# Attention units of 128 queries with 64-key windows in place of tiles of 64 queries with 96 keys, inside a fused attention and mixture-of-experts kernel

## The chip, the cores and the metric

The kernel runs on one core of one Trainium2 chip. The metric is device time in microseconds (us) of one launch. PE is TensorE (matmuls), DVE is VectorE, ACT is ScalarE, POOL is GpSimd, SP is the engine that issues all DMAs here.

## The reference

Chunked attention, then a gated MLP, then a soft mixture of experts, all in float32:

```
q, k, v: (4, 8, 768, 64); mem_k, mem_v: (4, 8, 8, 64)
for each chunk c of 32 queries:
    keys = 8 memory keys + keys from 16 before the chunk to 8 behind it, cut at the ends of the sequence
    scores = (q_c @ keys.T) / 8; a = softmax(scores, max subtracted, sum + 1e-9)
    out[c] = a @ values
x = out as (3072, 512)
h = x @ w_in (512 x 2048); g = h * sigmoid(h); x = g @ w_out
logits = x @ phi (32 slots); dispatch = softmax over all 3072 tokens; slot_input = dispatch.T @ x
slot_out = relu(slot_input @ w1[e]) @ w2[e] for 8 experts of 4 slots
result = softmax(logits over the slots) @ slot_out
```

## The kernel before

The 3072 tokens are worked on in seven blocks of 256, 512 x 5 and 256 tokens (TILES counts them in tiles of 64). In block b PE runs 16 chunks k of the MLP (pe_mlp, 12 matmuls of 128x128 weights by 512 tokens, or 256 in the two short blocks, into one of two h_ps buffers), and between the chunks it does the attention of the tokens of block b+1 and the mixture's sums of block b-1. So the attention of block 1 runs within block 0, and that of block 0 ahead of everything (the start). PE's order is written out by hand in pe_block; act_block and dve_block have the same steps for ACT and DVE, and each engine works its own list strictly in order, with semaphores between them.

A tile of attention is 64 queries of 8 heads. S_STEP gives the chunks behind which its steps start; T_LAG and V_LAG say how many chunks later the next steps come:

- S, pe_scores: 8 matmuls of 64 queries by the tile's 96 keys (88 around the two query chunks and 8 memory keys). dve_scores scales them, adds a mask of -3e38 for keys that a query may not see (masks, from PSUM to sc in SBUF), and takes the maximum. act_exp does 4 exponentials of 96 keys with the maximum as bias and the sum in the accumulator. dve_rinv takes the reciprocals, and POOL multiplies sc by them.
- T, pe_probs_T: 4 transposes to pt_ps; act_pt copies them to pt.
- V, pe_values: 8 matmuls of the values by pt into o_ps. dve_x splits the result into a high part (fp32r) and a low part, which are the MLP's input x.

The names of the other steps on PE: L is pe_logits (once per four chunks of the MLP), then pe_fold and D, pe_dispatch (64 matmuls of 32x32 weights, once per block, behind chunk 4, or 5 in the last block); pe_w2 and pe_w2_T run once in block 0. keep_busy matmuls fill waits of PE at the start and the end.

Behind a chunk, ACT does the tanh of the gate (act_tanh) and DVE multiplies (dve_g) and transposes (dve_gb). Chunk k waits for dve_g of chunk k-2. The weights w_in are split too: ACT makes the high half wh (act_wh), POOL (the first two DVE) the low half wl (low_part); eight pieces in all, and in block 0 the chunks 4, 8 and 12 wait for two more pieces each (wl_done). After the last block come the slots' MLP over 32 units of expert weights that SP streams in, and the output.

In the matmul groups of the trace a float32 matmul leaves two records, an fp32r one and a transpose one record. SP loads a tile's q and k (320 KB) and v (192 KB) into a ring of four.

Of the kernel before, what the change touches and what calls it, by code (L numbers as in the profile page):

```python
# [7 lines left out]
QT = 64  # L8
# [9 lines left out]
PAIRS = H // 2  # L18
QKW = PAIRS * QT + PAIRS * KEYS
LOADW = QKW + H * D  # L20
RING = 4
SB = 3
# [4 lines left out]
TILES = (4, 8, 8, 8, 8, 8, 4)  # L27
NB = len(TILES)
LAST = NB - 1
FIRST = [sum(TILES[:b]) for b in range(NB + 1)]  # L30
NT = FIRST[-1]
TOKS = [QT * t for t in TILES]
TMAX = max(TOKS)
BATCH_TILES = S // QT

S_STEP = (0, 1, 6, 7, 8, 9, 10, 11)
T_LAG, V_LAG = 2, 3
# [4 lines left out]
W_FIRST = (1, 2)  # L42
W_NEXT = (0, 1, 3, 4, 6, 7)
W_LOW_BEFORE = {4: (2, 3), 6: (4, 5), 7: (6,), 8: (7,)}


def tile_at(b, k, lag):

    if b == LAST or k - lag not in S_STEP[:TILES[b + 1]]:
        return None  # L50
    return FIRST[b + 1] + S_STEP.index(k - lag)


def moe_program(nc, qk, v, w_in, w_outT, w_out, phi, w1, w2, out):
# [5 lines left out]
    with ExitStack() as ctx:  # L60
# [30 lines left out]
        masks = at("masks", R, [128, 3, KEYS])  # L91
        sc = at("sc", R + 288, [128, SB, PAIRS, KEYS])
        pt = at("pt", R + 288 + 1152, [KEYS, PAIRS, 2 * QT])
        row_stats = at("row_stats", R + 1952, [128, 4, SB, PAIRS])
        ring = at("ring", R + 2000, [128, RING, LOADW])
        assert 2000 + RING * LOADW <= 4 * HALF_W
        nmax, rsum, rinv = (row_stats[:, i, :, :] for i in range(3))
# [18 lines left out]
        def x_of(b):  # L116
            return x_short if TILES[b] == 4 else (x_even, x_odd)[b % 2]

        def gt_of(b, k):
            if b == 0:  # L120
                return gT_short[:, k, :] if k < 2 * GT_RING else acc_short[:, k - 2 * GT_RING, :]
            return gT[:, (NCH * (b - 1) + k) % GT_RING, 0:TOKS[b]]

        def gb_of(b, k):
            if TILES[b] == 4:
                return gB_short[:, k, :]
            return gB[:, k + 16 if b % 2 and k < 8 else k, :]

        def gb_groups(b, i, j):

            rows, cols = slice(32 * i, 32 * i + 32), slice(32 * j, 32 * j + 32)
            if TILES[b] == 4:
                return gB_short[rows, :, cols]
# [13 lines left out]

        qk_in = [sem(f"qk_in{t}") for t in range(RING)]
        v_in = [sem(f"v_in{t}") for t in range(RING)]
# [23 lines left out]
        def q_of(n, p, h2):  # L173
            return ring[64 * h2:64 * h2 + 64, n % RING, p * QT:(p + 1) * QT]

        def k_of(n, p, h2):
            o = PAIRS * QT + p * KEYS
            return ring[64 * h2:64 * h2 + 64, n % RING, o:o + KEYS]

        def half_of(p, h2):  # L180

            return h2 ^ (p % 2)

        def v_of(n, h):
            return ring[0:KEYS, n % RING, QKW + h * D:QKW + (h + 1) * D]

        def s_of(n):
            return sx_ps if n >= TILES[0] or n % 2 == 0 else lpu_ps
# [6 lines left out]
        def pe_scores(pe, n, dispatched=0):  # L195
            pe.wait_ge(qk_in[n % RING], 16 * (n // RING + 1))
            if n >= TILES[0]:
                pe.wait_ge(sc_done, n)
            elif n >= 2:
                pe.wait_ge(sc_done, n - 1)  # L200
            if dispatched:
                pe.wait_ge(acc_done, 4 * dispatched - 1)
            for p in range(PAIRS):
                for h2 in range(2):
                    r, cols = 64 * half_of(p, h2), slice(p // 2 * KEYS, (p // 2 + 1) * KEYS)
                    last = nc.tensor.matmul(s_of(n)[r:r + 64, p % 2, cols], q_of(n, p, h2), k_of(n, p, h2),  # L206
                                            start=True, stop=True)
# [716 lines left out]
```

## Time and profile before

| | us |
|---|---|
| median of 3 runs | 522.82 (521.74 to 528.11) |
| profiled execution | 526.73 |
| its span, first to last instruction | 524.9 |
| PE busy | 492.9 (94%) |
| DVE busy | 306.2 (58%) |
| ACT busy | 181.2 (35%) |
| POOL busy | 55.8 (11%) |

Busy time says how long an engine had an instruction under way. For PE it is modelled, and a PE that is always busy can still spend its time in short gaps between unlike matmuls. A stage's length is read from the starts of its instructions. The execution and its span differ by 1.8 us; the profiled execution was 3.9 us longer than the median of the runs.

### The profile page before, as it was taken

What the parts mean: (1) busy time and instruction counts of PE and PEld (TensorE: products, weight loads), DVE (VectorE), ACT (ScalarE), POOL (GpSimd) and SP (SyncE); (2) the same over time, 40 slices, a digit from 0 to 9 for tenths busy, and PEclk for the clock granted to TensorE, in tenths of its full rate; (3) what the DMA queues carried; (4) which work ended last, traced back from release to release, by engine and by line L of the source; (5) the groups of instructions that cost most, each with busy time, mean ns of one, the idle gap of its engine ahead of it and who ended that gap; (6) DMA issues with size and microseconds to landing.
All of it is one profiled execution on the core that took longest, in us unless ns stands there. A gap on an engine that the chain in (4) does not pass through costs nothing.

```text
span 524.9 us, 11609 instructions
## 1 busy us (share of the span) xinstructions
PE 492.9 (94%) x4794; PEld 350.0 (67%) x4794; DVE 306.2 (58%) x733; ACT 181.2 (35%) x591; POOL 55.8 (11%) x65
## 2 busy tenths in 40 slices
PE   5779899999999999999999999999999989999972
PEld 4668677777776777776777767776677769643541
DVE  3546745756576676475665767656765466561222
ACT  3555623345333254341642505524132112110112
POOL 2154400011100011010110101101010000000000
PEclk9799999999999999999999999999999999999978
DMA  8587621202312013111132010341005659989997
GB/s 270 179 278 242 199 84 40 83 1 81 121 41 81 2 66 123 57 44 39 42 121 81 23 59 23 101 131 70 2 1 198 259 197 420 426 345 423 425 345 253
DMA packets 25125, 78.42 MB, mean 149 GB/s; under 512 B 2416, under 2 KB 8688, under 8 KB 19440
## 3 DMA queue, kind: packets, MB, share of 16 engines
q1 hardware_dynamic: 25072, 77.67, 41.1%
q8 instruction: 38, 0.62, 0.5%
q14 instruction: 15, 0.12, 0.1%
HBM read 71.37 MB, written 6.29 MB: 148 GB/s over the span
## 4 chain that ended last, share of the span: by engine, by line
PE 85%; DMA 8%; DVE 2%; ACT 2%; issue 1%; POOL 1%; SPq 1%; DVEq 0%; ACTq 0%
PE h_ps L243 52%; PE o_ps L225 6%; DMA unit<-w 5%; PE pt_ps L215 5%; PE lpu_ps L257 5%; PE sx_ps L206 4%; PE lpu_ps L277 3%; PE sx_ps L277 2%; DMA w_stage<-w_in 2%; PE h_ps L857 1%; PE h_ps L794 1%; DMA ring<-qk 1%; PE pt_ps L794 1%; ACT sc L352 1%; PE lpu_ps L265 1%
## 5 line engine op out<-in xcount | busy, mean ns | idle before, releaser
L243 PE MATMUL h_ps<-x_odd,wh 128*128 128x512 f32 x384 | 130.7, 402 | 0.0
L340 ACT ACTIVATE gT<-h_ps 128x512 f32<-128x512 f32 (+1 forms) x108 | 57.7, 534 | 154.9 <-PE h_ps L243 145.1
L352 ACT ACTIVATE sc<-sc,row_stats 128x96 f32<-128x96 f32 x192 | 69.7, 364 | 79.1 <-DVE row_stats L395 79.1
L422 DVE SCALAR_TENSOR_TENSOR gT<-gT,h_ps 128x512 f32<-128x512 f32 (+1 forms) x108 | 65.9, 610 | 53.1 <-ACT gT L340 51.4
L243 PE MATMUL h_ps<-x_even,wh 128*128 128x512 f32 x256 | 87.6, 403 | 0.0
L243 PEld LDWEIGHTS h_ps<-x_odd,wh 128*128 128x128 f32 x384 | 72.1, 188 | 23.1 <-issue 5.4
L243 PE MATMUL h_ps<-x_odd,wl 128*128 128x512 f32 x192 | 75.1, 391 | 0.0
L669 POOL TENSOR_TENSOR sc<-sc,row_stats 128x384 f32<-128x384 f32 x48 | 39.7, 827 | 324.8 <-DVE row_stats L402 324.8
L243 PEld LDWEIGHTS h_ps<-x_even,wh 128*128 128x128 f32 x256 | 48.0, 188 | 14.9 <-issue 3.4
L432 DVE STREAM_TRANSPOSE gB<-gT 128x512 f32<-128x512 f32 x80 | 56.6, 708 | 1.3
L243 PE MATMUL h_ps<-x_short,wh 128*128 128x256 f32 x256 | 54.3, 299 | 1.5 <-DVE gT L422 1.5
L243 PE MATMUL h_ps<-x_even,wl 128*128 128x512 f32 x128 | 50.1, 391 | 0.0
L243 PEld LDWEIGHTS h_ps<-x_short,wh 128*128 128x128 f32 x256 | 42.9, 197 | 7.6 <-issue 3.8
L243 PEld LDWEIGHTS h_ps<-x_odd,wl 128*128 128x128 f32 x192 | 36.1, 188 | 6.2
L225 PEld LDWEIGHTS o_ps<-pt,ring 96*64 96x64 f32 x768 | 27.2, 141 | 16.7 <-issue 16.3
L346 ACT COPY pt<-pt_ps 96x512 f32<-96x512 f32 x48 | 27.8, 579 | 29.0 <-PE pt_ps L215 24.2
L215 PE MATMUL pt_ps<-ident,sc 128*96 128x128 f32 x192 | 31.1, 286 | 6.2 <-POOL sc L669 4.2
L243 PE MATMUL h_ps<-x_short,wl 128*128 128x256 f32 x128 | 37.0, 289 | 0.0
L352 ACT ACTIVATION_READ_ACCUMULATOR sc<-sc,row_stats 128x1 f32 x192 | 35.9, 187 | 0.0
L225 PE MATMUL o_ps<-pt,ring 96*64 96x64 f32 x768 | 33.8, 232 | 1.9 <-DVE x_short L411 1.1
L215 PEld LDWEIGHTS pt_ps<-ident,sc 128*96 128x96 f32 x192 | 20.2, 129 | 19.1 <-issue 12.0
L389 DVE SCALAR_TENSOR_TENSOR sc<-sx_ps,masks 128x192 f32<-128x192 f32 x92 | 28.4, 350 | 5.9 <-PE sx_ps L206 5.9
(143 smaller groups left out, 567.8 us busy)
## 6 DMA issues: line engine op xcount, KB each, us to landing
unit<-w SPq DMA_DIRECT2D x32, 1024.0 KB, 11.4
ring<-qk SPq DMA_DIRECT2D x48, 320.0 KB, 3.1
ring<-v SPq DMA_DIRECT2D x48, 192.0 KB, 3.2
w_stage<-w_in SPq DMA_DIRECT2D x4, 1024.0 KB, 10.0
wot<-w_outT SPq DMA_DIRECT2D x4, 1024.0 KB, 8.1
unit<-w_out SPq DMA_DIRECT2D x4, 1024.0 KB, 5.7
out<-unit SPq DMA_DIRECT2D x4, 1024.0 KB, 7.4
out<-unit SPq DMA_DIRECT2D x2, 512.0 KB, 5.5
```

What stands on the lines that cost most here:

```text
L215: last = nc.tensor.transpose(pt_ps[0:KEYS, p * 128:(p + 1) * 128], sc[:, n % SB, p, :], ident[:])
L225: last = nc.tensor.matmul(o_ps[64 * h2:64 * h2 + 64, p * QT:(p + 1) * QT], v_of(n, 2 * p + h2), pt[:, p, QT * half_of(p, h2):QT * half_of( ...
L243: last = nc.tensor.matmul(h_ps[k % 2][:, 0:TOKS[b]], w[:, n, kc, q * 128:(q + 1) * 128], x[:, lo, kc, 0:TOKS[b]], start=(kc == 0 and w is ...
L257: last = nc.tensor.matmul(lp_ps[32 * q:32 * q + 32, 0:TOKS[b]], w2c[:, q, 32 * n:32 * n + 32], gt_of(b, 4 * n + q), start=(n == 0), stop=( ...
L277: last = nc.tensor.matmul(u_ps[i][32 * c:32 * c + 32, :], eB[32 * i:32 * i + 32, 32 * j:32 * j + 32], gb_groups(b, i, j), start=(r == 0), ...
L340: nc.scalar.activation(gt_of(b, k), h_ps[k % 2][:, 0:TOKS[b]], ACT.Tanh, scale=0.5).then_inc(tanh_done, 1)
L346: nc.scalar.copy(pt[:], heads(pt_ps[0:KEYS, :])).then_inc(pt_done, 1)
L352: last = nc.scalar.activation(sc[:, i, p, :], sc[:, i, p, :], ACT.Exp, bias=nmax[:, i, p:p + 1], accum_out=rsum[:, i, p:p + 1])
L389: last = nc.vector.scalar_tensor_tensor(out=sc[:, i, c::2, :], in0=s_of(n)[:, c, 0:2 * KEYS].rearrange("p (a k) -> p a k", a=2), scalar=D ...
L422: nc.vector.scalar_tensor_tensor(out=gt_of(b, k), in0=gt_of(b, k), scalar=1.0, in1=h_ps[k % 2][:, 0:TOKS[b]], op0=ALU.add, op1=ALU.mult).t ...
L432: nc.vector.transpose(gb_of(b, k), gt_of(b, k)).then_inc(gb_done, 1)
L669: nc.gpsimd.tensor_tensor(p, p, rinv[:, n % SB, :].unsqueeze(2).to_broadcast([128, PAIRS, KEYS]), ALU.mult).then_inc(p_done, 1)
```

## The change

- The work comes in units of 128 queries (24 of them; UNITS is 2, 4 x 5, 2). A query chunk of 32 gets its own window of 64 keys, WIN = 16 + 32 + 8 + 8, which it sees in full. The memory keys are placed within the 96 keys (key_order) so that both windows of a tile are contiguous. The masks are gone; at the two ends of a sequence dve_scores writes -3e38 over the columns outside it in PSUM.
- S is 32 matmuls of 32 queries by 64 keys, 8 of them at different places of the array in a row. DVE takes the maximum straight from PSUM and scales it; ACT takes 8 exponentials of 64 keys from PSUM with scale, bias and accumulator, 4 behind one chunk's tanh and 4 behind the next. The POOL multiply is over 512 columns instead of 384, and there is one per unit.
- T is 4 transposes of 128x128; ACT copies in two halves into pt, whose other places stay zero. V is 16 matmuls with 128 rows of weights, since v is loaded once per window (twice the overlap).
- ACT makes the high part of x (act_x), DVE the low part.
- There is one pause per four chunks: T behind chunk 0, 4, 8, 12 (1, 5, 9, 13 in block 0), then V, L and S behind the next one (V and S in block 0).
- q and k are loaded per unit (two in flight, freed by S), v per unit (three in flight). In the last block the gate's buffers are halved and doubled in number, D is behind chunk 6 and the logits behind 9, 10 and 13.
- In block 0 the pieces of wh are at chunks 2, 3, 6, 7, 10, 11 (W_NEXT), two per pause, and POOL's wl goes ahead of the multiply of the same unit (W_LOW_BEFORE). The start has longer keep_busy runs and includes the exponentials of unit 2.

```diff
+WIN = LEFT + CHUNK + RIGHT + NMEM
-TILES = (4, 8, 8, 8, 8, 8, 4)
-S_STEP = (0, 1, 6, 7, 8, 9, 10, 11)
-T_LAG, V_LAG = 2, 3
-W_NEXT = (0, 1, 3, 4, 6, 7)
-W_LOW_BEFORE = {4: (2, 3), 6: (4, 5), 7: (6,), 8: (7,)}
+UNITS = (2, 4, 4, 4, 4, 4, 2)
+W_NEXT = {2: 2, 3: 3, 6: 4, 7: 5, 10: 6, 11: 7}
+W_LOW_BEFORE = {3: (2, 3), 4: (4, 5), 5: (6, 7)}
+def values_at(b, n):
+    if b >= LAST or UNITS[b + 1] == 2 and n % 2 == 0:
         return None
+    return FIRST[b + 1] + (n if UNITS[b + 1] == 4 else n // 2)
+def scores_at(b, n):
+    return values_at(b, n + 1) if n < 3 else values_at(b + 1, 0)
+def pause(b):
+    return 2 if b == 0 else 1
...
+            for t in range(2):
+                for c in range(2):
+                    for p in range(PAIRS):
+                        for h2 in range(2):
+                            a, r = place_of(p, h2)
+                            at = (2 * t + c) * WIN
+                            last = nc.tensor.matmul(s_of(u)[32 * r:32 * r + 32, a, at:at + WIN], q_of(u, t, c, p, h2),
+                                                    k_of(u, t, c, p, h2), start=True, stop=True)
...
         def pe_block(pe, b):
             for k in range(NCH):
                 pe_mlp(pe, b, k)
+                n, at_pause = k // 4, k % 4 == pause(b)
+                if k % 4 == pause(b) - 1 and values_at(b, n) is not None:
+                    pe_probs_T(pe, values_at(b, n))
...
+                if at_pause and values_at(b, n) is not None:
+                    pe_values(pe, values_at(b, n))
...
+        def act_exp(act, u, a):
+            if a == 0:
+                act.wait_ge(nmax_done, u + 1)
+            for g in range(4 * a, 4 * a + 4):
+                last = nc.scalar.activation(sc[:, u % SB, g, :], by_window(u)[:, a, g - 4 * a, :], ACT.Exp, scale=D ** -0.5,
+                                            bias=rmax[:, u % SB, g:g + 1], accum_out=rsum[:, u % SB, g:g + 1])
...
+        def act_x(act, u):
+            hi, lo = unit_x(u)
+            act.wait_ge(o_mm, u + 1)
+            nc.scalar.copy(hi, heads(o_ps)).then_inc(xh_done, 1)
...
         def act_block(act, b):
             for k in range(NCH):
                 if b == 0 and k in W_NEXT:
-                    act_wh(act, 2 + W_NEXT.index(k))
+                    act_wh(act, W_NEXT[k])
                 act_tanh(act, b, k)
+                if k % 4 == pause(b) + 1 and scores_at(b, n) is not None:
+                    act_exp(act, scores_at(b, n), 1)
+                if k % 4 == pause(b) - 1 and values_at(b, n) is not None:
+                    act_pt(act, values_at(b, n))
+                if at_pause and values_at(b, n) is not None:
+                    act_x(act, values_at(b, n))
...
+                if at_pause and scores_at(b, n) is not None:
+                    act_exp(act, scores_at(b, n), 0)
```

PE in block 1, behind chunk 9, before: V (o_ps), L (w2c), T (pt_ps) and S (sx_ps) of three different tiles, between two chunks of the MLP (h_ps).

```order
L243 MATMUL h_ps<-x_odd,wh 128x512
L225 MATMUL o_ps<-pt,ring 64x64 x8
L257 MATMUL lpu_ps<-gT,w2c 32x512 x4
L215 MATMUL pt_ps<-ident,sc 96x128 x4
L206 MATMUL sx_ps<-ring 64x96 x8
L243 MATMUL h_ps<-x_odd,wh 128x512
```

The same place after the change.

```order
L261 MATMUL h_ps<-x_odd,wh 128x512
L242 MATMUL o_ps<-pt,v_sb 64x64 x16
L275 MATMUL lpu_ps<-gT,w2c 32x512 x4
L219 MATMUL sx_ps<-qk_sb 32x64 x32
L261 MATMUL h_ps<-x_odd,wh 128x512
```

The transposes have moved to a break of their own one chunk earlier; behind chunks 10 and 11, where before V, T and S of the next tiles follow each time, nothing stands any more.

ACT in block 0, chunks 4 to 7 before: wh is a piece of the weights, gT the tanh, sc the exponentials.

```order
L340 ACTIVATE gT<-h_ps 128x256 x2
L368 CAST wh<-w_stage 128x1024
L340 ACTIVATE gT<-h_ps 128x256
L352 ACTIVATE sc,row_stats<-sc,row_stats 128x96 x4
L368 CAST wh<-w_stage 128x1024
L340 ACTIVATE gT<-h_ps 128x256
L352 ACTIVATE sc,row_stats<-sc,row_stats 128x96 x4
```

ACT at chunks 5 to 7 after the change (x_odd is the high part of x, written by act_x).

```order
L375 COPY pt<-pt_ps 64x16x32 x2
L408 CAST wh<-w_stage 128x1024
L365 ACTIVATE gT<-h_ps 128x256
L394 CAST x_odd<-o_ps 128x4x128
L382 ACTIVATE sc,row_stats<-sx_ps,row_stats 128x64 x4
L408 CAST wh<-w_stage 128x1024
L365 ACTIVATE gT<-h_ps 128x256
L382 ACTIVATE sc,row_stats<-sx_ps,row_stats 128x64 x4
```

The second wh piece of a pause stands behind x and the first four exponentials of the unit scored in that pause; before, the pieces 2 and 3 stood at chunks 0 and 1, well ahead of chunk 4.

## Rows read from the trace of the kernel before

**Rows 1.** The page, part 1: PE's busy time.

```profile
PE 492.9 (94%) x4794; PEld 350.0 (67%) x4794; DVE 306.2 (58%) x733; ACT 181.2 (35%) x591; POOL 55.8 (11%) x65
```

**Rows 2.** Stretches: block 0; block 2; block 6; expert weights. Clock, DMA share last.

```profile
28.40:81.40 53.00, 45.94 (x528) 37.25 (x517) 30.40 (x89) 26.40 (x93) 18.33 (x13) 0.94 0.60 198
...
150.00:218.60 68.60, 68.60 (x646) 48.57 (x650) 45.25 (x105) 26.70 (x92) 6.62 (x8) 1.00 0.19 63
...
414.00:448.00 34.00, 32.45 (x355) 26.50 (x354) 20.73 (x49) 7.20 (x19) 0.00 (x0) 1.00 0.78 313
...
466.00:506.00 40.00, 36.10 (x450) 17.12 (x450) 12.30 (x33) 4.42 (x8) 0.00 (x0) 0.99 0.98 392
```

**Rows 3.** The chain that ended last, in order of time: start, us, what.

```profile
479.25 26.78 DMA unit<-w
```

**Rows 4.** Waits of PE in block 0: us in total, times, longest.

```profile
PE pt_ps L215 <- POOL sc L669: 4.2, 2, 3.5
```

**Rows 5.** Timeline of PE around S of one tile: start, us, what.

```profile
218.17 0.39 PE L243 MATMUL h_ps<-x_odd,wh 128*128 128x512 f32 x1
218.49 0.56 PE L206 MATMUL sx_ps<-ring 64*64 64x96 f32 x16
218.98 0.50 PE L243 MATMUL h_ps<-x_odd,wh 128*128 128x512 f32 x1
```

**Rows 6.** Timeline of PE behind chunk 10 of block 2: V, T, S, next chunk.

```profile
194.07 0.69 PE L225 MATMUL o_ps<-pt,ring 96*64 96x64 f32 x16
194.69 0.64 PE L215 MATMUL pt_ps<-ident,sc 128*96 128x128 f32 x4
195.26 0.56 PE L206 MATMUL sx_ps<-ring 64*64 64x96 f32 x16
195.75 0.50 PE L243 MATMUL h_ps<-x_even,wh 128*128 128x512 f32 x1
```

**Rows 7.** Timeline of PE in D of block 2, and the chunk behind it.

```profile
166.40 0.62 PE L277 MATMUL sx_ps<-gB,eB 32*32 32x512 f32 x2
166.41 0.62 PE L277 MATMUL lpu_ps<-gB,eB 32*32 32x512 f32 x2
...
167.50 0.63 PE L277 MATMUL lpu_ps<-gB,eB 32*32 32x512 f32 x2
167.53 0.62 PE L277 MATMUL sx_ps<-gB,eB 32*32 32x512 f32 x2
...
170.78 0.50 PE L243 MATMUL h_ps<-x_even,wh 128*128 128x512 f32 x1
```

**Rows 8.** Groups of instructions on ACT, POOL, DVE: busy, mean ns, idle before.

```profile
L352 ACT ACTIVATE sc<-sc,row_stats 128x96 f32<-128x96 f32 x192 | 69.7, 364 | 79.1 <-DVE row_stats L395 79.1
L346 ACT COPY pt<-pt_ps 96x512 f32<-96x512 f32 x48 | 27.8, 579 | 29.0 <-PE pt_ps L215 24.2 <-PE o_ps L225 4.8
L368 ACT CAST wh<-w_stage 128x1024 fp32r<-128x1024 f32 x8 | 8.3, 1039 | 1.9 <-DMA w_stage<-w_in 1.9
...
L669 POOL TENSOR_TENSOR sc<-sc,row_stats 128x384 f32<-128x384 f32 x48 | 39.7, 827 | 324.8 <-DVE row_stats L402 324.8
L416 POOL TENSOR_TENSOR wl<-w_stage,wh 128x1024 fp32r<-128x1024 f32 x6 | 14.2, 2369 | 11.0 <-ACT wh L368 11.0
...
L395 DVE TENSOR_REDUCE row_stats<-sc 128x4 f32<-128x384 f32 x48 | 26.6, 553 | 1.6
```

**Rows 9.** Timeline of PE: keep_busy at the start, and pe_w2 in block 0.

```profile
7.61 1.16 PE L794 MATMUL h_ps<-ident,fold 128*128 128x128 f32 x8
...
69.26 3.64 PE L287 MATMUL lpu_ps<-wot,part 128*32 128x512 f32 x32
```

**Rows 10.** Timeline of PE behind its longest wait.

```profile
38.43 1.12 PE L225 MATMUL o_ps<-pt,ring 96*64 96x64 f32 x16
39.49 1.09 PE L215 MATMUL pt_ps<-ident,sc 128*96 128x128 f32 x4
```

**Rows 11.** One stretch of block 0 behind that wait; granted clock third from the end.

```profile
38.40:40.60 2.20, 2.20 (x23) 2.02 (x23) 0.96 (x3) 0.38 (x1) 2.19 (x1) 0.50 0.12 33
```

More of the change, by code:

```diff
@@ L88, in moe_program @@
         cmax, csum, crinv = (csoft[:, i, :] for i in range(3))
[L91 to L97, printed above, removed]
+        sc = at("sc", R, [128, SB, 2 * PAIRS, WIN])
+        pt = at("pt", R + 1024, [128, 4 * PAIRS, QT])
+        row_stats = at("row_stats", R + 2048, [128, 3, SB, 2 * PAIRS])
+        qk_sb = at("qk_sb", R + 2112, [128, QK_RING, 2, QKW])
+        v_sb = at("v_sb", R + 2112 + QK_RING * 2 * QKW, [128, V_RING, 2, H * D])
+        assert 2112 + QK_RING * 2 * QKW + V_RING * 2 * H * D <= 4 * HALF_W
+        rmax, rsum, rinv = (row_stats[:, i, :, :] for i in range(3))
         x_odd = at("x_odd", R + 4 * HALF_W, [128, 2, KC, TMAX], fp32r)
@@ L201, in pe_scores @@
             if dispatched:
                 pe.wait_ge(acc_done, 4 * dispatched - 1)
[L203 to L207, printed above, removed]
-            last.then_inc(s_mm, 1)
-        def pe_probs_T(pe, n):
-            pe.wait_ge(p_done, n + 1)
-            if n:
-                pe.wait_ge(pt_done, n)
-            for p in range(PAIRS):
-                last = nc.tensor.transpose(pt_ps[0:KEYS, p * 128:(p + 1) * 128], sc[:, n % SB, p, :], ident[:])
-            last.then_inc(p_tr, 1)
@@ L342, in act_pt @@
-        def act_pt(act, n):
-            act.wait_ge(p_tr, n + 1)
-            if n:
-                act.wait_ge(o_mm, n)
-            nc.scalar.copy(pt[:], heads(pt_ps[0:KEYS, :])).then_inc(pt_done, 1)
-        def act_exp(act, n):
-            act.wait_ge(nmax_done, n + 1)
-            i = n % SB
-            for p in range(PAIRS):
-                last = nc.scalar.activation(sc[:, i, p, :], sc[:, i, p, :], ACT.Exp, bias=nmax[:, i, p:p + 1],
-                                            accum_out=rsum[:, i, p:p + 1])
-            last.then_inc(exp_done, 1)
+            r = NCH * (b - 1) + k
@@ new lines, in act_tanh, with act_pt @@
+            nc.scalar.activation(gt_of(b, k), h_ps[k % 2][:, 0:TOKS[b]], ACT.Tanh, scale=0.5).then_inc(tanh_done, 1)
+        def act_pt(act, u):
+            act.wait_ge(p_tr, u + 1)
+            if u:
+                act.wait_ge(o_mm, u)
+            else:
+                act.wait_ge(pt_zero, 1)
+            for c in range(2):
+                half = slice(64 * c, 64 * c + 64)
+                last = nc.scalar.copy(pt[half, :, c * CHUNK:(c + 1) * CHUNK], pt_ps[half, :].rearrange("p (j q) -> p j q", q=CHUNK))
+            last.then_inc(pt_done, 1)
@@ L506, in dve_block @@
                     dve_acc(dve, b - 1)
-        places = [(7, h_mm, NCH * LAST - NCH)] + [(i, o_mm, NT) for i in range(4)]
+        places = [(7, h_mm, NCH * LAST - NCH)] + [(i, o_mm, NUN) for i in range(4)]
         places += [(4, h_mm, NCH * LAST), (5, h_mm, NCH * LAST)]
@@ L662, in _ @@
                 pool.wait_ge(const_set, j + 2)
-            for n in range(NT):
+            for n in range(NUN):
                 for m in W_LOW_BEFORE.get(n, ()):
```

378 lines of the change are left out of this document (192 added, 186 removed).

## The prediction

> **What bounds the kernel now.** Three views, in this order. The page's first part has PE busy for 492.9 of 524.9 us [rows 1], so PE's own list sets the time, but an average does not say where. The stretches do: block 2 lasts 68.6 us with PE busy throughout at the full clock, DVE at 45.25 and ACT at 26.70 us [rows 2]. There what counts is PE's work and the gaps between unlike matmuls; a faster DVE is worth nothing. Block 0 is different: 53.0 us with 45.94 busy and a mean clock of 0.94. Its longest wait of PE is 3.5 us, for POOL's multiply of probabilities, which stood behind a piece of wl [rows 4]. Behind it the granted clock is 0.50, the level of 1.2 GHz [rows 11]. In block 6 PE is idle for 1.55 of 34.0 us. At the end the chain runs over DMA for 26.78 us [rows 3], the DMA engines being 98% busy from 466 to 506 us; those loads start when PE has finished earlier steps, so time won on PE ahead of block 6 moves them too and counts in full.
>
> **PE in a full block, step by step.** I call a pause's steps T, V, S, L and D as the code does.
>
> Breaks. With S alone, the last matmul of a chunk starts at 218.17, S at 218.49, the next chunk at 218.98 [rows 5]. The last matmul streams for 0.23 us (2.72 us per uninterrupted chunk by 12), so 0.09 is lost ahead of S; the first matmul behind a break takes 0.1 us longer than its neighbours. A break costs 0.2 us beside its content. Before, 15 of 16 chunks of a full block are followed by one; afterwards 9 (chunks 0, 1, 2, 4, 5, 8, 9, 12, 13). 6 x 0.2 = 1.2 us less.
>
> T. 194.69 to 195.26 is 0.57 us ahead of S [rows 6], 0.36 to 0.40 ahead of a chunk; the mean of 8 is 0.48, or 3.8 us per block. Afterwards four sets of four, with 128 columns for 96; nearest is a set of 128x128 transposes elsewhere in this trace at 0.46 us, so 1.8 us. 2.0 us less.
>
> V. 194.07 to 194.69 is 0.62 us for 8 matmuls, 16 records [rows 6]. Within it pairs start every 0.058 us, with 0.1 at the start and 0.15 at the end. A unit has 32 records: 0.1 + 15 x 0.058 + 0.15 = 1.13 us, in place of 1.24. 0.4 us less.
>
> S. This is the unknown price. Before, 0.49 us for 16 records of 96 keys, four at a time at the four places of 64x64. Afterwards 64 records of 64 keys, eight at a time. Low end: if only streaming counts, eight rounds of 0.058 and the ends, 0.65 us per unit. High end: D has 128 records of 32x32 places from 166.39 to 170.78 [rows 7], 0.034 us each, so 64 x 0.034 = 2.2 us. D also shows how it gets there: its first records start 0.007 us apart (two per row, rows 0.013 apart), later ones 0.017 apart (167.50 to 167.53 for two), with a gap of 0.19 us each 32 records. I take what D does as long as its queue is full, and the slower rate behind it: 32 records in four rounds, 0.11 + 3 x 0.058, then 32 x 0.017 = 0.54, and 0.26 for gap and ends, 1.1 us, against 2 x 0.49 before. 0.5 us more per block.
>
> Sum of a full block: -1.2 - 2.0 - 0.4 + 0.5 = -3.1, rounded with the restarts to -3.2 us. For blocks 1 to 4 that is -12.8, and -1.1 more since block 4 has three S instead of four. Block 5, with half the attention: 12 breaks become 7 (-1.0), T -1.0, V -0.2, S +0.3: -1.9.
>
> A rule speaks against this step. The Trainium skill (TensorEngine Tiling (Array Packing), Instruction Overhead) gives each small matmul some 60 cycles on trn2, and advises against tiling out of a dimension that is small already. At 2.4 GHz that is an estimate of 25 ns per record, 1.6 us for S. The trace has 7 and 17 ns between records of different places, so it does not agree for short runs. By the Trainium skill's figure the total would be near no change, since 21 units x 0.5 us take the whole gain.
>
> **Do the other engines keep up in a full block?** Take PE's S as ending at 0. DVE's maximum over 512 columns scales from 0.553 at 384 [rows 8] to 0.7, with the scaling 0.9 and the handover 0.2: 1.1. Four exponentials, 0.364 each [rows 8], 1.4: 2.5. The next chunk ends at 2.9 (with its fold 3.8), its tanh takes 0.6, the other four exponentials end at 5.0, the two DVE steps at 5.4, POOL's multiply (0.827 scaled by 512/384, 1.1) at 6.5. T is wanted behind the third chunk, at 8.3 or later. Its slack of 1.8 us is cover for all of ACT's added work, and x on ACT has the whole of the next chunk. Dropping the masks (0.35 us twice per tile) shortens DVE's list, which waits anyway: nothing. The larger v loads are hidden, with DMA at 0.19 in block 2 [rows 2]. No new wait, no gain.
>
> **Block 0.** Here the order of ACT makes a wait that was not there. From the start of T: T 0.46, chunk 1.5, V 1.1, S 1.1 end at 4.2. Maximum and scaling end at 5.4, exponentials (four) start at 5.6 and end at 7.0. Only then comes the second wh piece, 1.04 us [rows 8], to 8.0, since ACT works in order, and then POOL's wl, 2.37 [rows 8], to 10.4. The next chunk (4, 8 or 12) waits for that wl; its predecessor ended at 5.8. PE is idle for 4.6 us, with nothing beside it. Behind the ACT instruction stand also the tanh and the other exponentials; POOL's multiply is behind wl, but ends at 11.5, and T is wanted only at 13.5, behind two chunks of 1.5. So three periods of 13.5, 40.5 us.
>
> The first T of these: ACT bounds the start. First exponentials at 6.8 (as before; the q and k load is twice as large), 16 of them to 12.4. T waits for 20 keep_busy matmuls, 40 records at 0.145 [rows 9] = 5.8 us, to 15.3; the pt copies, 2 x 0.58 [rows 8] overlapping, 16.5; keep_busy and V 18.7; x, wh, pt 21.6; V of unit 1 22.8; x 24.7; maximum 25.6; eight exponentials 28.4; sums and multiply 29.9. Then 30 + 40.5 + 11.6 (T 0.5, w2 3.6 [rows 9], two chunks 3, V 1.1, S 1.1, transposes and logits 2.0, breaks 0.3) = 82.1, against 81.4 now [rows 2]. The low clock comes on top: after the 3.5 us wait of before, V took 1.06 instead of 0.62 and T 0.74 instead of 0.40 [rows 10], in all some 1.6 us. Three longer waits at 1.3 each, since part of the low stretch can fall into the wait: +4.0. Block 0 ends at 86.1: +4.7. Bounds: 0, if the wait is covered by less work ahead of wh than I count, and +9.
>
> **The last block and the tail.** D one chunk later, the ring of 12 buffers and the logits elsewhere: the transposes of dve_et still stand in front of a gate multiply, so the wait of 1.5 us stays; DVE's four sums now delay the gate behind D by some 0.6. +0.5. SP's queue for expert weights starts its long run at D, 1.4 us later; the DMA has about 2 us of air at 462 to 466, so it hides.
>
> **Sum.** -12.8 - 1.1 - 1.9 + 4.7 + 0.5 = -10.6 us. From the profiled execution, 526.73, that is 516.1; its runs' median is 3.9 us lower, 522.8, and I predict against that: 512.
>
> The Trainium skill (ScalarE: Activation LUTs, What ACT_TABLE_LOAD costs) gives 280 ns and 0.833 per element for an activation with a pointer as bias: 360 for 96 keys, and the row has 364, so it agrees. For 64 keys it is an estimate of 333, and block 0 and the start would be about 1 us shorter by it.
>
> **Rivals.**
> 1. Forecast: 512, between 509 and 516. Chance 0.42.
> 2. Block 0 costs nothing, or S runs near its low end. Without the +4.7: 507; with S at 0.65 as well, 21 units x 0.45 = 9.5 less, 498, but both together are unlikely. For it: four S records start within 0.02 us today. Against: the fixed order of ACT. About 507, chance 0.25.
> 3. A wait shows up in full blocks, or the low clock holds longer in block 0. If T waits 0.5 us per unit in 16 units, 8 us are gone: 520. Against it stands the slack of 1.8. Chance 0.19.
> 4. The other side: S is bound by its number of records all the way, as D is on average, at 2.2 us per unit. 21 units x 1.1 = 23 us more: 535. The gain is gone from 1.6 us per unit on, and it is 2% slower from 2.1. For it: twice as many records as before, and three quarters of D's run are at the slower rates. Against: V, S before and D's first 32 are far quicker. Chance 0.10, most of it below 2.1. The Trainium skill's estimate above (TensorEngine Tiling (Array Packing), Instruction Overhead) would put S at the first of these two points.
> 5. The change doesn't do what it says, the pauses being kept but lengthened by ring loads of q and k that come too late (two in flight, 640 KB each): about 522 to 535. Chance 0.04.
>
> **How the numbers follow.** A measurement of this kernel tells about 2%, 10.5 us, from no change: the line is at 512.4. Case 1 straddles it, slightly more below (0.23); with case 2 that is 0.48 for faster. Slower: 0.04 of case 4, 0.02 of case 5 and 0.02 of case 3: 0.08. Within 2%: 0.44. The range takes all of case 1, most of 2 and 3 and the lower part of 4: 503 to 521.
>
> **What would show it.** A full block of about 65.4 us instead of 68.6 with PE never idle; S of some 1.1 us between its start and the next chunk; T at 0.46, four per block. In block 0, three waits of PE of 4 to 5 us at chunks 4, 8 and 12, named after POOL's wl, with the clock at 0.50 behind each. The forecast is wrong if S takes 1.6 us or more, if T waits for POOL in full blocks, or if those three waits are absent or twice as long.

## The result, and the profile after

The changed kernel takes 504.39 us (median of four runs, 503.69 to 505.04) beside 524.17 for the kernel before on the same chip: a ratio of 0.962, interval 0.955 to 0.968. The forecast was 512, with 503 to 521 as its range. The sign is right, the time lies near the low end of the range, and the gain is nearly twice the one forecast. The profiled execution took 504.32 us (526.73 before, 2.6 above its median; so the profiles are 22.4 us apart and the medians 19.8). The page's first part, and then stretches of the changed kernel: block 0, block 2, block 6, and what follows the last block's matmuls.

```profile
PE 466.5 (93%) x5502; PEld 346.3 (69%) x5502; DVE 251.9 (50%) x508; ACT 182.6 (36%) x615; POOL 41.3 (8%) x41
```

```profile
22.70:83.90 61.20, 45.32 (x652) 39.60 (x652) 24.48 (x57) 29.73 (x111) 18.37 (x10) 0.86 0.49 178
144.50:207.90 63.40, 63.40 (x755) 47.27 (x754) 36.30 (x72) 26.84 (x95) 4.14 (x5) 1.00 0.22 76
...
392.60:427.00 34.40, 32.56 (x355) 26.43 (x354) 20.30 (x49) 7.20 (x19) 0.00 (x0) 1.00 0.89 361
427.00:502.50 75.50, 61.67 (x705) 33.05 (x703) 27.23 (x62) 10.68 (x21) 0.00 (x0) 0.96 0.96 380
```

PE is 26.4 us less busy than in [rows 1], with 708 more matmul records. A full block is still PE without a gap, now 63.4 us for 68.6 in [rows 2]. Block 0 went the other way: 61.2 us with 15.9 of them idle and a mean clock of 0.86.

Cut at the first MLP matmul of each block, the trace gives where the 22.4 us of span went:

```
                   before   after    change   forecast
start               26.49   22.72     -3.8  } together
block 0             54.82   61.21     +6.4  } +4.7
block 1             65.78   60.57     -5.2     -3.2
block 2             68.58   63.43     -5.15    -3.2
block 3             68.58   63.43     -5.15    -3.2
block 4             68.58   62.62     -6.0     -4.3
block 5             61.17   58.60     -2.6     -1.9
block 6             33.9    34.4      +0.5     +0.5
behind the matmuls  77.0    75.5      -1.4      0
sum                                  -22.4    -10.6
```

The waits of PE in block 0, as in [rows 4], are those forecast:

```profile
PE h_ps L261 <- POOL wl L458: 13.9, 3, 4.7
PE pt_ps L228 <- POOL sc L721: 1.8, 1, 1.8
```

The first of the three, in order of time; "<-" in brackets names what ended the idle time:

```profile
34.23 1.05 ACT L408 CAST wh<-w_stage 128x1024 fp32r<-128x1024 f32 x1
...
35.36 2.34 POOL L458 TENSOR_TENSOR wl<-w_stage,wh 128x1024 fp32r<-128x1024 f32 x1 [2.36 <-ACT wh L408]
...
37.76 0.58 PE L261 MATMUL h_ps<-x_short,wh 128*128 128x256 f32 x1 [4.60 <-POOL wl L458]
...
42.59 0.60 PE L228 MATMUL pt_ps<-ident,sc 128*128 128x128 f32 x4
```

ACT converts its second piece of wh behind the four exponentials, POOL's piece of wl follows, and chunk 4 starts with its end. The granted clock in the three stretches around these waits, third number from the end, is 0.50, the level of 1.2 GHz:

```profile
35.20:42.00 6.80, 4.25 (x20) 4.25 (x21) 2.71 (x6) 1.93 (x11) 3.38 (x2) 0.50 0.92 367
52.20:55.60 3.40, 2.90 (x13) 2.91 (x14) 0.98 (x3) 0.00 (x0) 1.48 (x2) 0.50 0.97 380
65.90:72.70 6.80, 5.51 (x26) 5.51 (x27) 2.33 (x5) 0.67 (x3) 2.28 (x2) 0.50 0.00 1
```

In a full block, the break behind chunk 1 of block 2, timeline of PE (compare [rows 6]):

```profile
150.52 1.15 PE L242 MATMUL o_ps<-pt,v_sb 128*64 128x64 f32 x32
151.60 1.06 PE L275 MATMUL lpu_ps<-gT,w2c 128*32 128x512 f32 x8
152.60 0.86 PE L219 MATMUL sx_ps<-qk_sb 64*32 64x64 f32 x64
153.38 0.50 PE L261 MATMUL h_ps<-x_even,wh 128*128 128x512 f32 x1
```

V takes 1.08 us (151.60 less 150.52). S, whose price was the large unknown, takes 0.78 for its 64 records, less than two of the old S. The last chain over the DMA engines has nearly the length that it had in [rows 3]; it starts 21 us earlier:

```profile
458.32 26.43 DMA unit<-w
```

### The profile page after: what moved, and what is told of

Same layout as the page of the kernel before. It is cut to its first block, busy times and chain, and to the rows that moved or that the text cites. A ratio compares the mean times of both kernels' runs of the same rounds, so it can differ in the third digit from the quotient of the medians.

```text
span 502.5 us, 12654 instructions
## 1 busy us (share of the span) xinstructions
PE 466.5 (93%) x5502; PEld 346.3 (69%) x5502; DVE 251.9 (50%) x508; ACT 182.6 (36%) x615; POOL 41.3 (8%) x41
## 4 chain that ended last, share of the span: by engine, by line
PE 81%; DMA 6%; ACT 5%; DVE 4%; POOL 2%; issue 1%; DVEq 0%; SPq 0%; ACTq 0%
PE h_ps L261 51%; DMA unit<-w 5%; PE lpu_ps L275 5%; PE o_ps L242 4%; PE lpu_ps L295 3%; PE sx_ps L219 3%; PE h_ps L832 2%; PE pt_ps L228 2%; PE sx_ps L295 2%; ACT wh L408 2%; PE h_ps L890 1%; POOL wl L458 1%; ACT sc L382 1%; PE pt_ps L832 1%; ACT pt L375 1%
## 5 line engine op out<-in xcount | busy, mean ns | idle before, releaser
L261 PE MATMUL h_ps<-x_odd,wh 128*128 128x512 f32 x384 | 126.9, 400 | 0.0
L382 ACT ACTIVATE sc<-sx_ps,row_stats 128x64 f32<-128x64 f32 x184 | 55.2, 318 | 50.5 <-DVE row_stats L441 50.5
L261 PE MATMUL h_ps<-x_short,wh 128*128 128x256 f32 x256 | 57.1, 312 | 15.9 <-POOL wl L458 13.9
L721 POOL TENSOR_TENSOR sc<-sc,row_stats 128x512 f32<-128x512 f32 x24 | 25.0, 1043 | 314.6 <-DVE row_stats L448 314.6
L382 ACT ACTIVATION_READ_ACCUMULATOR sc<-sx_ps,row_stats 128x1 f32 x184 | 38.8, 211 | 0.0
L242 PEld LDWEIGHTS o_ps<-pt,v_sb 128*64 128x64 f32 x768 | 24.4, 138 | 7.5 <-issue 6.9
L375 ACT COPY pt<-pt_ps 64x512 f32<-64x512 f32 x48 | 27.7, 577 | 4.0 <-PE pt_ps L228 3.5
L242 PE MATMUL o_ps<-pt,v_sb 128*64 128x64 f32 x768 | 27.6, 225 | 0.4 <-issue 0.4
L261 PEld LDWEIGHTS h_ps<-x_even,wl 128*128 128x128 f32 x128 | 24.1, 188 | 5.0 <-issue 0.5
L261 PEld LDWEIGHTS h_ps<-x_short,wl 128*128 128x128 f32 x128 | 27.1, 212 | 0.3 <-issue 0.2
L219 PEld LDWEIGHTS sx_ps<-qk_sb 64*32 64x32 f32 x1472 | 16.4, 107 | 15.2 <-issue 14.4
```

Source lines behind the costliest of these rows:

```text
L219: last = nc.tensor.matmul(s_of(u)[32 * r:32 * r + 32, a, at:at + WIN], q_of(u, t, c, p, h2), k_of(u, t, c, p, h2), start=True, stop=True)
L242: last = nc.tensor.matmul(o_ps[64 * h2:64 * h2 + 64, at:at + QT], v_sb[:, u % V_RING, t, h * D:(h + 1) * D], pt[:, (2 * a + t) * 4 + r, :] ...
L261: last = nc.tensor.matmul(h_ps[k % 2][:, 0:TOKS[b]], w[:, n, kc, q * 128:(q + 1) * 128], x[:, lo, kc, 0:TOKS[b]], start=(kc == 0 and w is ...
L375: last = nc.scalar.copy(pt[half, :, c * CHUNK:(c + 1) * CHUNK], pt_ps[half, :].rearrange("p (j q) -> p j q", q=CHUNK))
L382: last = nc.scalar.activation(sc[:, u % SB, g, :], by_window(u)[:, a, g - 4 * a, :], ACT.Exp, scale=D ** -0.5, bias=rmax[:, u % SB, g:g + ...
L721: nc.gpsimd.tensor_tensor(p, p, rinv[:, n % SB, :].unsqueeze(2).to_broadcast([128, 2 * PAIRS, WIN]), ALU.mult).then_inc(p_done, 1)
```

## The experiments

The first four runs separate block 0 from the full blocks, and S and the breaks within those. Edits are against the changed kernel.

**The wh pieces earlier.** The pieces 2 to 7 of wh go ahead of the exponentials that delayed them.

```
-W_NEXT = {2: 2, 3: 3, 6: 4, 7: 5, 10: 6, 11: 7}
+W_NEXT = {0: 2, 1: 3, 4: 4, 5: 5, 8: 6, 9: 7}
```

> The changed kernel with one table altered: in block 0 the two pieces of wh of each group stand at chunks 0, 1, 4, 5, 8, 9 instead of 2, 3, 6, 7, 10, 11, ahead of the pause whose exponentials they stood behind. Theory A: the three waits of 4.6 to 4.7 us for POOL's wl come from ACT's order alone. Then they are gone, the half clock behind them too, and what is late next is T, which waits about 1 us for POOL's multiply: each of three periods falls from about 15 to about 10 us, block 0 from 61.2 to about 46 us, the time from 504.4 to about 490. Rival B: POOL cannot do two pieces of wl (4.8 us) and a multiply in the period in time, and T takes over the wait: block 0 at 56 us or more, the time at 499 or more.

Measured: 489.47 us (488.96 to 489.98), ratio to the kernel before 0.934, interval 0.931 to 0.938. Block 0 and block 3 in the stretches, and the waits of PE in block 0:

```profile
22.75:68.38 45.63, 40.41 (x653) 34.06 (x653) 22.04 (x57) 28.87 (x111) 18.27 (x10) 1.00 0.65 239
192.35:255.78 63.43, 63.43 (x756) 47.29 (x755) 35.70 (x68) 26.84 (x95) 4.18 (x5) 1.00 0.23 76
```

```profile
PE pt_ps L228 <- POOL sc L721: 3.5, 4, 1.7
PE h_ps L261 <- DVE gT L464: 1.5, 3, 0.6
```

Block 0 became 15.6 us shorter, and the start and blocks 1 to 6 did not move; only the stretch behind the last block's matmuls was 1.2 us longer, of which more below. Idle time fell by 10.7 us (15.9 to 5.2), and the same matmuls were busy 4.9 us less, the clock being 1.00 throughout instead of 0.86. So two thirds of what the order had cost were idle time and one third the low clock. The cause of block 0's loss is shown: the order of ACT's list.

**S issued twice.**

```
-            for t in range(2):
+            for t in (0, 1, 0, 1):
```

> The changed kernel with all 32 score matmuls of a unit issued twice over (the same result written again), 64 records more per unit. Theory A: S is bound by eight places that stream side by side, as its 0.79 us per 64 records says, and the second round costs the same without the ends: +0.7 us per unit, a full block at 66.2 instead of 63.4, 21 units and the start +15 us, about 519 us. Rival B: the first records only profit from a full queue, and from there on records start 0.017 us apart: +1.1 us per unit, a full block at 67.8, about 528 us. Rival C: as D on average, 0.034 per record: +2.2 us per unit, about 550 us.

Measured: 522.10 us (one run). The break behind chunk 1 of block 2:

```profile
160.11 1.07 PE L275 MATMUL lpu_ps<-gT,w2c 128*32 128x512 f32 x8
161.11 1.48 PE L219 MATMUL sx_ps<-qk_sb 64*32 64x64 f32 x128
162.52 0.50 PE L261 MATMUL h_ps<-x_even,wh 128*128 128x512 f32 x1
```

128 records take 1.41 us where 64 took 0.78: 0.63 for the second 64, 0.010 us each. A full block is 65.9 to 66.0 us, 2.5 more or four times that, close to theory A's 66.2; B and C fall. The forecast had 1.1 us for S, and the fourth rival 2.2; both were too high. The total is 3 us above theory A's 519. 3.4 us of it lie in the start (26.1 us for 22.7), where the first T began at 17.03 for 13.62: 0.9 us for each of the two doubled S ahead of it, 0.3 for a later first S, and a wait of PE within the second S for which the profile names no releaser:

```profile
11.80 0.73 PE L219 MATMUL lpu_ps<-qk_sb 64*32 64x64 f32 x49 [1.35 <-issue]
```

**L in breaks of its own.** The logits move one chunk on, so three breaks per block are added and no work.

```
-                if 0 < b < LAST and k in (5, 9, 13):
+                if 0 < b < LAST and k in (6, 10, 14):
```

> The changed kernel with L of blocks 1 to 5 one chunk later, in a break of its own, and nothing else changed. Theory A: a break costs 0.2 us beside its content, so 15 more breaks give +3.3 us, a full block at 64.1 instead of 63.4 us. Rival B: the breaks that went away were worth nothing by themselves and the gain is all in T, V and S: no change. Rival C: the gate's tanh behind chunks 6, 10 and 14 now waits for L to free its buffer, and PE waits in turn: more than 5 us longer.

Measured: 508.08 us (507.22 to 510.04), ratio 0.971, interval 0.967 to 0.974. A full block is 64.06 us: 0.63 more for three breaks, 0.21 each, beside the 0.2 of the forecast. Theory A holds: the price of a break is right where logits stand in it.

**The maximum issued twice.** DVE has 0.69 us more per unit, right behind S.

```
-            nc.vector.tensor_reduce(m..., AX.X, ALU.max, negate=True).then_inc(max_done, 1)
-            dve.wait_ge(max_done, u + 1)
+            for twice in range(2):
+                nc.vector.tensor_reduce(m..., AX.X, ALU.max, negate=True).then_inc(max_done, 1)
+                dve.wait_ge(max_done, 2 * u + 1 + twice)
```

> The changed kernel with DVE's maximum over a unit's scores taken twice, 0.7 us more of DVE per unit. Theory A: in full blocks DVE's work is covered, so the masks that were dropped were worth nothing there: a full block stays at 63.4 us. In block 0 and the start it is on the chain to the exponentials, wh and wl: +0.7 in each of three periods and twice at the start, in all +3 to +4 us, about 508 us. Rival B: the relief of DVE is a part of the gain everywhere: +0.7 per unit, 17 us, about 521 us.

Measured: 510.46 us (one run). Block 0 and block 2 in the stretches, and the waits of PE:

```profile
23.30:89.85 66.55, 47.27 (x653) 41.44 (x653) 27.72 (x62) 29.93 (x111) 18.34 (x10) 0.85 0.45 168
150.30:213.60 63.30, 63.30 (x756) 47.20 (x755) 39.04 (x76) 26.65 (x95) 4.13 (x5) 1.00 0.22 76
```

```profile
PE h_ps L261 <- POOL wl L459: 15.9, 3, 5.4
```

In the full block 2.7 us more of DVE change nothing, as the forecast had it. In block 0 the maximum stands in the chain maximum, exponentials, wh, wl, and the three waits are 2.0 us longer in all. Of the 5.3 us that the block lost, 3.4 are idle time and 1.9 a longer busy time of the same matmuls (47.27 for 45.32) at the lower clock, which the expectation had left out.

Four more runs ask what bounds T and S, and whether the start hangs on PE.

**T issued twice.**

```
-            for j in range(4):
+            for j in (0, 1, 2, 3, 0, 1, 2, 3):
```

> Every T issues its four transposes twice. A set alone in a break adds 0.36 us to the two chunks around it, where the prediction had 0.46 for the set and 0.2 for the break. Theory A: the set's own time is all of it or more (four starts 0.11 to 0.12 us apart), and a break for transposes of 128x128 costs nothing beside it: each second set adds 0.43 to 0.47 us, a full block lasts 65.2 us instead of 63.4, and the whole takes about 514. Rival B: the break costs 0.2 us as the others do and the set only 0.16: each second set adds 0.16, a full block lasts 64.1, and the whole takes 508.

Measured: 514.26 us (one run). T and the chunk behind it in block 2:

```profile
150.67 1.03 PE L228 MATMUL pt_ps<-ident,sc 128*128 128x128 f32 x8
151.46 0.48 PE L261 MATMUL h_ps<-x_even,wh 128*128 128x512 f32 x1
```

From start to start 0.79 us for eight; the chunk step with T in it grows by 0.44, though the next step with V is 0.04 shorter, and a full block is 64.97 us (+1.54). Theory A holds in its numbers (65.2 and 514 expected), and rival B falls. But the 0.36 us that both start from is not all that a T alone costs. In the changed kernel, T behind chunk 8 of block 2, and the first and the last matmul of chunk 9:

```profile
181.68 0.60 PE L228 MATMUL pt_ps<-ident,sc 128*128 128x128 f32 x4
182.04 0.48 PE L261 MATMUL h_ps<-x_even,wh 128*128 128x512 f32 x1
...
184.67 0.39 PE L261 MATMUL h_ps<-x_even,wh 128*128 128x512 f32 x1
```

T takes 0.36 us (182.04 less 181.68), and the twelve matmuls behind it start over 2.63 us, where those of a chunk that follows a chunk start over 2.49 (eleven twelfths of 2.72). So a T alone costs 0.50 in all, and of that a set is worth 0.40 (0.44 less the 0.04 that the next step was shorter) to 0.44; the break beside it is worth 0.1 at most and not 0.2. The forecast had charged 0.46 + 0.2.

**S in another order.** The four matmuls of a head follow each other at one place of the array.

```
-            for t in range(2):
-                for c in range(2):
-                    for p in range(PAIRS):
-                        for h2 in range(2):
+            for p in range(PAIRS):
+                for h2 in range(2):
+                    for t in range(2):
+                        for c in range(2):
```

> The same 32 matmuls per S in another order: the four of one head, which write the same place of 64 rows by 32 columns of the array, follow each other, where the change goes round all eight places. Theory A: S is bound by the places. A record of 64 keys holds its place for about 0.06 us (V: a pair every 0.058), and eight places work beside each other, which gives 64 x 0.06 / 8 = 0.5 us and the ends. In a row of eight records on one place only the last overlaps the next place: 56 x 0.058 + 8 x 0.01 = 3.3 us, 2.5 more per unit, a full block of 73 us and about 555 in all. Rival B: S is bound by the starts of its records (0.011 us each), whatever their place: nothing changes, 504 us.

Measured: 542.24 us (one run). S and the chunk behind it:

```profile
154.83 2.40 PE L219 MATMUL sx_ps<-qk_sb 64*32 64x64 f32 x64
157.17 0.50 PE L261 MATMUL h_ps<-x_odd,wh 128*128 128x512 f32 x1
```

The same 64 records take 2.34 us instead of 0.78. Rival B falls: the order over the places matters. But theory A's size was off too, 1.56 more per unit and not 2.5 (full block 69.54, and 542 in all for 555). The starts of single records show why: in a row they lie 0.026 and 0.030 us apart by turns, 0.056 for the two records of one matmul. So a record of 64 keys holds its place for some 0.028 us, half of what I read from V's pairs.

**Half the keys.** From the fourth unit on each matmul of S has 32 keys.

```
+            w = 32 if u > UNITS[0] + 1 else WIN
...
-  matmul(s_of(u)[32 * r:32 * r + 32, a, at:at + WIN], q_of(...), k_of(...), ...)
+  matmul(s_of(u)[32 * r:32 * r + 32, a, at:at + w], q_of(...), k_of(...)[:, 0:w], ...)
```

> From the fourth unit on, each matmul of S computes only the first 32 of its 64 keys; the others keep the scores of earlier units, so the output is not the reference's. Theory A: S is bound by how long its places are held by streaming, so the part that grows with the number of keys halves: 0.25 to 0.3 us less per unit, a full block of 62.3 instead of 63.4, and about 499.5 in all. Rival B: S is bound by its number of records, and neither the blocks nor the whole change by more than 1 us: 504.

Measured: 505.28 us (one run). S and the chunk behind it:

```profile
154.30 0.76 PE L220 MATMUL sx_ps<-qk_sb 64*32 64x32 f32 x64
154.99 0.50 PE L262 MATMUL h_ps<-x_even,wh 128*128 128x512 f32 x1
```

0.69 us for 0.78: 0.09 to 0.10 less per unit, a full block of 62.91. Neither theory holds as put. Starts of single records of S, in us from its first:

```
                          changed kernel     32 keys        in a row
record 9                  0.08               0.05           0.36
record 32                 0.24               0.17           1.09
record 64                 0.64               0.57           2.19
apart, first 32           7 ns, and a round  5 to 7 ns      28 ns mean
                          of 8 every 56 ns                  within a head
apart, records 40 to 59   8.2 ns             8.3 ns         as above
```

The first 32 records come in rounds of eight, one round every 0.056 us: four matmuls at four places, each of which holds its place for two records of 0.028. The next four matmuls go to the four other places and still start only with the next round. So in this stretch four places work beside each other and not eight, as theory A of the run before had it; why the others wait, no run separates. With 32 keys the rounds are shorter. The second 32 start one per 8 ns in their middle and one per 17 ns at both ends, whatever the keys, so they gain nothing. For 64 keys both limits come to 7 or 8 ns per record, which is why S is cheap in the order that goes round the places. The total is not lower than that of the changed kernel, because block 0 was 2.6 us longer in this run (its mean clock was 0.84, with 3.4 us more at 0.50, from 27.44 on) while the full blocks won 0.5 each.

**A shorter start.** With the wh pieces early, also the third run of keep_busy is shortened.

```
-            keep_busy(20, h_ps[0])
+            keep_busy(12, h_ps[0])
```

> The pieces 2 to 7 of wh are issued one chunk or two earlier, as in wh_early, and the third run of keep_busy at the start has 12 matmuls instead of 20. Theory A: the first T of the start waits for nothing but these matmuls (POOL's multiply had ended at 11.6 us, T began at 13.65), so the first chunk of block 0 begins 1.9 us earlier, at 20.8 instead of 22.7, and everything behind it with it: 487.6 us. Rival B: the start hangs on ACT's list or on the arrival of w_in, or the shorter run of matmuls lets the clock fall, so the first chunk begins at 22 us or later, or some stretch of block 0 runs at a granted clock of 0.50: 489 us or more.

Measured: 486.09 us (485.97 to 488.44), ratio to the kernel before 0.927, interval 0.923 to 0.930. The start of PE:

```profile
9.31 2.94 PE L832 MATMUL h_ps<-ident,fold 128*128 128x128 f32 x24
12.10 0.60 PE L228 MATMUL pt_ps<-ident,sc 128*128 128x128 f32 x4
...
21.20 0.39 PE L261 MATMUL h_ps<-x_short,wh 128*128 128x256 f32 x1 [0.94 <-DVE x_short L453]
```

T begins 1.5 us earlier than at 13.62, and the first chunk too, at 21.20 for 22.75. The eight matmuls left out were worth 1.8 us (2.94 for 4.73), and the second S stood 0.2 to 0.3 later in this run. So theory A holds with 1.5 for 1.9: at the start PE waited for its own filling work. Block 0 takes 45.67 us, at the full clock as before. It is 3.4 us faster than the kernel with the wh pieces early alone; of these the 1.5 are shown, and the rest lies in the stretch behind the last block's matmuls.

Two more runs ask how much cover ACT's added work has in the full blocks. "again" is a new semaphore.

**All exponentials issued twice.**

```
+            for n in range(1):
+                for g in range(4 * a, 4 * a + 4):
+                    last = nc.scalar.activation(...)
+                last.then_inc(again, 1)
+                act.wait_ge(again, 2 * u + a + 1)
             for g in range(4 * a, 4 * a + 4):
```

> Each group of four exponentials of 64 keys is issued twice, the second time once the first has ended: ACT's work grows by some 1.35 us per group (4 x 0.29 and the handover). Theory A: ACT's added work is hidden in full blocks by a slack; in the changed kernel POOL's multiply ends 1.9 us ahead of the T that needs it in three pauses of a block and 2.8 us ahead in the first. The first group now pushes the tanh back by 0.7 us and the second ends 2.2 us later than before, so T waits 0.3 us in three pauses: a full block of 64.3 us for 63.4. In block 0 and at the start there is no such slack: the wh pieces stand behind the first group (1.35 us each of three times) and 16 exponentials more stand ahead of the first T (4 to 5 us): 517 in all. Rival B: the units' chain sets the full blocks' time as it is, so all 2.7 us per unit show: 74 us per full block, 555 in all.

Measured: 530.58 us (one run). All waits of PE from 163 to 229 us, which is block 2:

```profile
PE lpu_ps L295 <- issue: 1.5, 1, 1.5
```

A full block took 64.92 to 65.16 us. T waited nowhere; the steps with T alone grew by 0.04 us at most places and 0.2 at a few. The 1.4 us went where no theory had looked, ahead of D. D needs eB and the kept logits, and they hang on the exponentials through DVE's list: the sums of the unit (L446) wait for its last exponential, the maximum of the dispatch (L483) stands behind them, ACT's exponential of dispatch (L399) waits for that, and DVE's transposes for this one. In the changed kernel the last of these transposes ends at 162.55 and D starts at 163.12:

```profile
158.27 0.17 DVE L446 TENSOR_SCALAR row_stats<-row_stats 128x8 f32<-128x8 f32 x1 [0.49 <-ACT sc L382]
...
158.60 0.64 DVE L483 TENSOR_REDUCE stats<-lpu_ps 128x1 f32<-128x512 f32 x1
...
159.85 0.69 ACT L399 ACTIVATE part<-lpu_ps,stats 128x512 f32<-128x512 f32 x1 [1.62 <-DVE stats L485]
...
161.30 1.25 DVE L493 STREAM_TRANSPOSE logits<-lpu_ps 32x128 f32<-32x128 f32 x4
...
163.12 0.61 PE L295 MATMUL lpu_ps<-gB,eB 32*32 32x512 f32 x1
```

The sum came out too low by 13.6 us (530.58 for 517), mostly in block 0 and the block behind it, which took 65.5 us (+5.0). Block 0 took 72.3 us, +11 and not +4. Its three waits for wl grew to 17.6 us in all, as expected, but T behind chunk 1 waited 4.4 us for POOL's multiply instead of 1.8, and the mean clock of the block was 0.81 for 0.86.

**The second group issued three times.**

```
+            for n in range(2 * a):
+                for g in range(4 * a, 4 * a + 4):
+                    last = nc.scalar.activation(...)
+                last.then_inc(again, 1)
+                act.wait_ge(again, 2 * u + n + 1)
             for g in range(4 * a, 4 * a + 4):
```

> Only the second group of four exponentials of a unit, which stands behind the tanh, is issued, three times, each once the one ahead has ended: 2.7 us more on ACT between scores and sums. Theory A: of this 1.9 us are hidden in three pauses of a full block and 2.7 in the first, so T waits 0.8 us three times: a full block of 65.8 us for 63.4, with waits of PE for POOL's multiply in blocks 1 to 4 of about 10 us in all; the start is 4 to 5 us longer, block 0 about the same: 519 in all. Rival B: the slack is larger than counted (another T is waited for), so full blocks stay within 0.3 us of 63.4. Rival C: there is no slack, and full blocks take 74 us.

Measured: 541.20 us (one run). Waits of PE in blocks 2 to 5, from 160 to 398 us:

```profile
PE lpu_ps L295 <- issue: 8.4, 4, 2.1
PE pt_ps L228 <- POOL sc L727: 5.8, 9, 0.7
```

T waits 0.65 us nine times; the step with it is 0.86 longer, for 0.8 expected. So T's slack of 1.9 us is as counted. Again it was D that made the sum wrong: 2.1 us each time, the 2.7 us added less D's 0.6. Full blocks took 68.0 to 69.6 us and the whole 22 us more than expected. Block 2 is 1.6 us longer than block 3, since 3.4 us right behind D's wait ran at the granted clock of 0.50 in it, as in block 4. The tightest cover of a full block is D's 0.6 us and not T's 1.9. The slack of T in order of time, in the changed kernel: POOL's multiply has ended at 179.78, and T starts at 181.68.

```profile
178.74 1.04 POOL L721 TENSOR_TENSOR sc<-sc,row_stats 128x512 f32<-128x512 f32 x1 [18.93 <-DVE row_stats L448]
```

## Why the prediction was right, and where it was off

**What bounds the kernel.** Right. PE's own list sets the time in blocks 1 to 5. DVE's list fell by 54 us and was worth nothing there, as the doubled maximum shows from the other side.

**Breaks, 0.2 each.** Right for L (0.21), the only kind that a run tested by itself. Too high for T alone: four transposes of 128x128 between chunks of 128x128 cost 0.50 us, the slower chunk behind them taken in, and the forecast had 0.66. Three times per full block, 0.5 us.

**V.** 1.08 us for the 1.13 worked out from pairs of 0.058: 0.2 us per block.

**S.** This term was mis-sized. The step that failed is "the slower rate behind it: 32 x 0.017". D's records start that far apart in [rows 7], but they have 512 columns on places of 32x32; most of the second half of S runs at 8 ns per record, half of that. The rate took 0.17 us too much, and the 0.26 for gap and ends, of which 0.14 is left, another 0.12. S took 0.78 us against 1.1, four times per block, 1.3 us. Together with T and V that is 2.0 us of cheaper work per full block, and 1.95 were seen (5.15 for 3.2).

The low end of the forecast (0.65, streaming alone) was nearer than the value taken. The forecast took the 60 cycles of the Trainium skill (TensorEngine Tiling (Array Packing), Instruction Overhead) per record, an estimate of 1.6 us for S; the measurement, 0.78 and 0.010 us for each further record, decides against that for small matmuls that go round different places. The page gives them per matmul, and S has 32: an estimate of 0.8 us, beside which the trace has 0.78, and 0.63 for 32 more. At one place, 0.037 us per record is what the run in a row shows, 2.34 us for S where two of the old ones took 0.98, and there the advice against fine tiling would have held.

**Block 0.** The mechanism and its price are right: three waits of 4.60, 4.59 and 4.70 us for wl, against 4.6. The period from T to T was 15.0, 14.4 and 15.5 us, 14.8 with the forecast's share of the low clock. What was off is its beginning: T at 27.59 and not 30. The forecast let keep_busy run for 5.8 us, at [rows 9]'s 0.145 per record; the forty records took 4.73 at 0.118, since that row's 1.16 us for eight records also hold the last record's own length and are too short to divide. Exponentials of 64 keys last 0.318 us on average and follow each other every 0.29, where 0.35 was used. With both, the first T came at 13.62 and not 15.3, which is 1.7 of the 2.4 us. The start itself became 3.8 us shorter: before the change PE waited there as the first rows show; afterwards only as the last two do:

```profile
PE lpu_ps L206 <- DMA ring<-qk: 2.6, 1, 2.6
PE pt_ps L215 <- ACT pt L346: 2.0, 1, 2.0
PE o_ps L225 <- DVE x_short L411: 1.1, 1, 1.1
```

```profile
PE sx_ps L219 <- issue: 0.5, 1, 0.5
PE o_ps L242 <- issue: 0.4, 1, 0.4
```

Start and block 0 together are 2.6 us longer, for 4.7 forecast. The Trainium skill (ScalarE: Activation LUTs, What ACT_TABLE_LOAD costs) gives an estimate of 333 ns for 64 keys; the rows have 302 to 356, 318 on average.

**Blocks 5 and 6.** Block 5 had the same cheaper T and S (0.7 us more), block 6 came as forecast.

**Behind the matmuls.** Forecast 0, measured -1.4. The granted clock there was 0.96 for 0.94. This stretch took 76.8 us at 0.92 with the wh pieces early and 74.6 at 0.94 with the shorter start, though both run the same instructions there. So the difference is probably variation, in the clock among other things, and no effect of the change; it was not tested by itself.

**The slack in full blocks.** T's slack was forecast at 1.8 us and is 1.9. But the forecast named only T as the one that waits. D's chain over ACT and DVE has 0.6, and the change would have lost time there had the second group of exponentials ended more than 0.6 us later. The prediction was right by less than it thought.

**Luck.** The medians are 19.8 us apart where the sum gave 10.6, 9.2 us off, and from 512 down to the end of the range there are only 9. Full blocks, start and block 0 all erred to the same side. The time lies in the range, 1.4 us from its end, because the kernel before took 524.17 us in this comparison and the forecast had started from 522.8.

**The rivals.** The second (507: block 0 free, or S near its low end) came nearest to the time, by its S half and not by block 0; the first, 509 to 516, missed it. The case that S is bound by its records at 2.2 us fell. So did the wait in full blocks, and the ring loads: q and k never arrived late in blocks 1 to 6, and the wait of 2.6 us that the kernel before had for its ring at the start is gone. The only wait of PE in blocks 1 to 6 is 1.8 us for the gate of block 6.

## What to carry to other kernels

Price many small matmuls by how long each holds its place and by how far apart their records start, and take both from rows of the same size of matmul. Order them so that consecutive ones go to different places: the same 32 matmuls took 0.78 us in one order and 2.34 in another.

When work becomes coarser, look at the engines that work in order next to the path. Here six pieces of wh, placed a chunk or two late in ACT's list, gave away 15.6 us of 61, and a table of six numbers brought them back.

A slack is that of the tightest waiter. Before calling added work hidden, list everybody that waits for that engine, also those that wait over a third one. Price a break by the chunk behind it too.

## What was unexpected of the hardware

A pass of four 128x128 transposes between two chunks costs 0.50 us, 0.14 of it in the chunk behind it; each set issued again costs 0.40 to 0.44. So its break is worth 0.1 us at most, where a break for logits at places of 32 columns is worth 0.21 (a full block of 64.06 us for 63.43).

Records of S that go round eight places start 7 ns apart in its first half and mostly 8 ns in its second, and one place takes a record of 64 columns each 28 ns. The 56 ns round of the first half is what four places need for two records each; halving the columns shortened it and left the 8 ns.

The low clock is not proportional to the wait. Around the wait of 4.6 us behind chunk 7 the granted clock was 0.50 for 3.4 us, around those of 4.6 and 4.7 behind chunks 3 and 11 for 6.8 us each, and the mean clock of block 0 was 0.86 with three such waits and 1.00 when the longest was 1.7 us. With the second group issued three times, PE waited 2.1 us ahead of D in each of the blocks 2 to 5, and the clock fell to 0.50 for 3.4 us behind two of the four waits.
